# One PSUM copy per group product, joined by a DMA and GpSimd, in a float32 attention and MLP kernel

## The reference, cut to what matters

```
# q, k, v: (2, 8, 768, 64)   proj: (64, 6)
q_bits = (einsum('bhsd,dk->bhsk', q, proj) > 0)          # k_bits likewise
q_bucket = sum(q_bits * 2 ** arange(6), axis=-1)
mask = q_bucket[..., :, None] == k_bucket[..., None, :]
scores = where(mask, q @ k.T / 8, -1e9)
attn = exp(scores - max(scores)); attn = attn / (sum(attn) + 1e-9)
x = (attn @ v) transposed to (1536 tokens, 512)
h = x @ w_in1;  x = (P(h) / (Q(h) + 1e-6)) @ w_out1      # d_ff 2048, P cubic, Q quadratic
h = x @ w_in2;  out = (h - tanh(h)) @ w_out2
```

## Time and profile before

| | |
|---|---|
| time, median of 3 runs | 791.07 us (790.76 to 792.19) |
| the profiled execution's own time | 794.7 us |
| its span, first to last instruction | 792.9 us |
| TensorE busy | 771.3 us, 97% |
| VectorE busy | 554.0 us, 70% |
| ScalarE busy | 476.0 us, 60% |
| GpSimd busy | 127.3 us, 16% |
| mean granted TensorE clock | 0.993 of full speed |

### The profile page before, as it was taken

How to read it: one execution, slowest core, us unless ns; L and a number is a source line. 1 busy time by engine, 2 the same in 40 slices (tenths; PEclk the granted TensorE clock), 3 DMA queues, 4 the chain that set the end, 5 groups by cost and what they waited for, 6 DMA issues and landing times.

```text
span 792.9 us, 11860 instructions
## 1 busy us (share of the span) xinstructions
PE 771.3 (97%) x3840; PEld 645.7 (81%) x3840; DVE 554.0 (70%) x894; ACT 476.0 (60%) x922; POOL 127.3 (16%) x112
## 2 busy tenths in 40 slices
PE   5979999999999999999999999999999999999998
PEld 3879899989998777877888888888888888888886
DVE  4859999999997999999888988965432322223222
ACT  5859889888887778887666767654432222222221
POOL 5334533543548200000000000000000000000000
PEclk9989999999999999999999999999999999999999
DMA  5766768768563520000000032330000100001001
GB/s 116 157 167 154 163 163 175 172 152 175 120 171 114 159 94 0 1 2 1 0 1 15 26 107 83 103 92 3 0 1 1 53 1 1 0 1 54 0 1 54
DMA packets 64603, 56.54 MB, mean 71 GB/s; under 512 B 31664, under 2 KB 50352, under 8 KB 64560
## 3 DMA queue, kind: packets, MB, share of 16 engines
q1 hardware_dynamic: 62848, 55.52, 28.4%
q10 hardware_dynamic: 1712, 0.46, 0.3%
HBM read 29.57 MB, written 3.19 MB: 41 GB/s over the span
## 4 chain that ended last, share of the span: by engine, by line
PE 75%; DVE 16%; issue 3%; DMA 2%; POOL 2%; SPq 1%; ACT 1%; DVEq 0%; POOLq 0%; ACTq 0%
PE acc L722 28%; PE h_ps L693 27%; PE slot L232 5%; PE turn_ps L354 5%; PE pv_ps L314 4%; PE pv_ps L316 3%; DVE sqr L828 2%; DVE row_min L505 2%; DVE pol L849 2%; DVE pol L841 1%; DVE pt_lo L552 1%; DVE pol L860 1%; DVE pol L835 1%; DVE wout_lo L889 1%; DVE g_lo L873 1%
## 5 line engine op out<-in xcount | busy, mean ns | idle before, releaser
L693 PE MATMUL h_ps<-x_hi,win_lo 128*128 128x512 f32 x384 | 151.6, 395 | 0.0
L693 PE MATMUL h_ps<-x_lo,win_hi 128*128 128x512 f32 x384 | 151.4, 394 | 0.0
L693 PE MATMUL h_ps<-x_hi,win_hi 128*128 128x512 f32 x384 | 151.2, 394 | 0.0
L743 ACT ACTIVATE g_hi<-pol 128x512 fp32r<-128x512 f32 x96 | 60.8, 634 | 129.5 <-PE acc L722 105.2
L873 DVE TENSOR_TENSOR g_lo<-pol,g_hi 128x512 fp32r<-128x512 f32 x96 | 65.9, 687 | 101.2 <-ACT g_hi L743 101.0
L552 DVE TENSOR_TENSOR pt_lo<-turn_ps,pt_hi 128x384 fp32r<-128x384 f32 x192 | 98.0, 551 | 11.2 <-ACT pt_hi L457 9.6
L457 ACT ACTIVATE pt_hi<-turn_ps 128x384 fp32r<-128x384 f32 x192 | 84.0, 490 | 23.7 <-PE turn_ps L354 22.7
L505 DVE TENSOR_REDUCE row_min<-slot 128x1 f32<-128x768 f32 x96 | 90.7, 944 | 7.1 <-PE slot L232 7.1
L433 ACT ACTIVATE E<-slot,row_min 128x768 f32<-128x768 f32 x96 | 87.3, 909 | 2.8 <-DVE row_min L505 2.8
L693 PEld LDWEIGHTS h_ps<-x_lo,win_hi 128*128 128x128 f32 x384 | 72.2, 188 | 17.0
L693 PEld LDWEIGHTS h_ps<-x_hi,win_hi 128*128 128x128 f32 x384 | 72.2, 188 | 16.7
(11 more groups left out here) (105 smaller groups left out, 1364.9 us busy)
## 6 DMA issues: line engine op xcount, KB each, us to landing
win_raw<-in_moe_w_in SPq DMA_DIRECT2D x32, 256.0 KB, 3.1
wout_raw<-in_moe_w_out SPq DMA_DIRECT2D x32, 256.0 KB, 2.8
q_nat<-in_q SPq DMA_DIRECT2D x16, 192.0 KB, 3.5
v_nat<-in_v SPq DMA_DIRECT2D x8, 384.0 KB, 5.4
scale<-softmax_scale SPq DMA_DIRECT2D x16, 192.0 KB, 3.3
qA<-q_hi SPq DMA_DIRECT2D x15, 192.0 KB, 2.5
qB<-q_hi SPq DMA_DIRECT2D x15, 192.0 KB, 2.9
qB<-q_lo SPq DMA_DIRECT2D x15, 192.0 KB, 3.2
```

The lines of the kernel that those rows point to most:

```text
L693: mm = eng.matmul(h_ps[t % 4][:, :], w[:, ws], columns(x, kt, c), start=kt + n == 0, stop=kt == KT - 1 and n == 2)
L743: eng.activation(g_hi[:, t % TEMPS, :], pol[:, t % TEMPS, :], ACT.Copy).then_inc(mlp_sems["g_hi"], 1)
```

## The change

- v's parts are placed so that head e's result always has its hi product on the partitions where head e's x belongs: hi in columns 64e to 64e+63, lo in the other half.
- One copy takes all 128 partitions of `pv_ps` to a new tile `x_raw[e]`: ScalarE for groups 0, 2 and 3, VectorE for group 1. The next group's product waits for that copy only.
- A new DMA per head, `shift`, moves the 64 rows of `x_raw[e]` that lie on the wrong partitions into `x_pair` (64 rows of 768 float32, 192 KB). A new GpSimd add, `pool_add`, adds the other 64 rows. A copy out waits until the same half of `x_raw` was added in the pair before.
- SyncE: shift(p-1, 1) stands between copy_split(p+1, 0) and scale_out(p, 0). scale_in(p, 0) moves behind copy_hot(p+1, 1), and shift(p, 0) follows it.
- GpSimd: pool_add(p, 0) stands in step 11, behind the split of q and ahead of that of k; pool_add(p-1, 1) stands in front of the multiply of `pool_x`. Of the weight tiles, two are split ahead of the last pair's steps and the others behind them, in the order in3, in4 after in2 with the `out` tiles between.
- The one-hot products alternate: q half 0, k half 0, q half 1, k half 1. `dve_scale` of head 0 moves from step 4 to step 5.

```diff
-        POOL_TILES = ([("in", j) for j in range(EARLY_IN)] + [("out", j) for j in range(EARLY_OUT)]
-                      + LATE[:3])
+        POOL_TILES = [("in", 0), ("in", 1), ("in", 2), ("in", 3), ("out", 0), ("in", 4), ("out", 1),
+                      ("out", 2), ("in", 5)]
+        POOL_FIRST = 2
-        HOT_STEPS = {1: (0, 0), 2: (0, 1), 3: (1, 0), 4: (1, 1)}
+        HOT_STEPS = {1: (0, 0), 2: (1, 0), 3: (0, 1), 4: (1, 1)}
+        DVE_GROUP = 1
...
@@ def pe_pv
-                eng.wait_ge(sems["x_sum"], BIAS + GROUPS * p + c)
+                done, count = group_out(p, c - 1) if c else group_out(p - 1, GROUPS - 1)
+                eng.wait_ge(done, count)
...
-        def act_pv_low(eng, p, c):
+        def group_free(eng, p, c):
             eng.wait_ge(sems["pv"], BIAS + GROUPS * p + c + 1)
-            eng.wait_ge(sems["x_sum"], BIAS + GROUPS * p + c)
-            eng.activation(pv_low[:, :], pv_ps[D:2 * D, 0:HALF], ACT.Copy
-                           ).then_inc(sems["pv_low"], 1)
+            eng.wait_ge(sems["x_add"], BIAS + 2 * p - 1 + c // 2)
+
+        def act_out(eng, p, c):
+            if c != DVE_GROUP:
+                group_free(eng, p, c)
+                eng.activation(group_at(c), pv_ps[:, 0:HALF], ACT.Copy).then_inc(sems["out_act"], 1)
...
-        def dve_x_sum(eng, p, c):
-            e, hf = divmod(c, 2)
-            eng.wait_ge(sems["pv_low"], BIAS + GROUPS * p + c + 1)
-            if c == 0:
-                eng.wait_ge(sems["xn"], BIAS + p)
-            eng.tensor_tensor(x_pair[e * D:(e + 1) * D, hf * HALF:(hf + 1) * HALF],
-                              pv_ps[0:D, 0:HALF], pv_low[:, :], ALU.add
-                              ).then_inc(sems["x_sum"], 1)
+        def dve_out(eng, p, c):
+            if c == DVE_GROUP:
+                group_free(eng, p, c)
+                eng.tensor_copy(group_at(c), pv_ps[:, 0:HALF]).then_inc(sems["out_dve"], 1)
...
+        def pool_add(eng, p, e):
+            mine = slice(e * D, (e + 1) * D)
+            for c in (2 * e, 2 * e + 1):
+                done, count = group_out(p, c)
+                eng.wait_ge(done, count)
+            eng.wait_ge(loads[f"shift{e}"], 16 * (p + 1))
+            eng.sem_inc(loads["pool_here"], 1)
+            eng.tensor_tensor(x_pair[mine, :], x_pair[mine, :], x_raw[e][mine, :], ALU.add
+                              ).then_inc(sems["x_add"], 1)
...
@@ def pool_att
+            if last:
+                pool_split_tiles(eng, range(POOL_FIRST))
...
                 if n == 10 and turn:
                     pool_split_qk(eng, p + 2, 0)
+                if n == 11 and not last:
+                    pool_add(eng, p, 0)
             if last:
+                pool_split_tiles(eng, range(POOL_FIRST, len(POOL_TILES)))
+                pool_add(eng, p, 0)
+                pool_x(eng, p, sems["x_add"], BIAS + 2 * p + 1)
...
@@ SyncE
+                def shift(p, e):
+                    for c in (2 * e, 2 * e + 1):
+                        done, count = group_out(p, c)
+                        eng.wait_ge(done, count)
+                        here()
+                    eng.wait_ge(sems["xn"], BIAS + p)
+                    here()
+                    eng.dma_start(x_pair[e * D:(e + 1) * D, :], x_raw[e][D - e * D:2 * D - e * D, :]
+                                  ).then_inc(loads[f"shift{e}"], 16)
...
                     copy_split(p + 1, 0)
+                    if not is_zero(p):
+                        shift(p - 1, 1)
                     scale_out(p, 0)
                     load_v(p + 1)
                     copy_hot(p + 1, 0)
-                    scale_in(p, 0)
                     copy_split(p + 1, 1)
                     copy_hot(p + 1, 1)
+                    scale_in(p, 0)
+                    shift(p, 0)
                     scale_out(p, 1)
                     scale_in(p, 1)
...
@@ the last pair: weights, then
+                shift(PAIRS - 1, 0)
                 scale_out(PAIRS - 1, 1)
                 scale_in(PAIRS - 1, 1)
+                shift(PAIRS - 1, 1)
```

More of the change, by code:

```diff
@@ L67, in build @@
         "pe": ["pt", "pv", "scores0", "scores1", "aux"],
-        "act": ["pt_hi", "exp0", "exp1", "aux_act", "pv_low"],
-        "dve": ["rowmin", "sum", "recip", "aux_dve", "pt_lo", "x_sum"],
-        "pool": ["hi", "lo", "vhi0", "vhi1", "vlo0", "vlo1", "xn", "xhi", "xlo"],
+        "act": ["pt_hi", "exp0", "exp1", "aux_act", "out_act"],
+        "dve": ["rowmin", "sum", "recip", "aux_dve", "pt_lo", "out_dve"],
+        "pool": ["hi", "lo", "vhi0", "vhi1", "vlo0", "vlo1", "x_add", "xn", "xhi", "xlo"],
     }
@@ L143, in build @@
         row_inv = sb(att, "row_inv", [P, 2, T], F32)
-        pv_low = sb(att, "pv_low", [D, HALF], F32)
+        x_raw = [sb(att, f"x_raw{e}", [P, S], F32) for e in range(2)]
         x_pair = sb(att, "x_pair", [P, S], F32)
@@ L213, in exp_done, with group_out @@
             return sems[f"exp{m % 2}"], BIAS + p * T + m // 2 + 1
+        DVE_GROUP = 1
+        def group_out(p, c):
+            if c == DVE_GROUP:
+                return sems["out_dve"], BIAS + p + 1
+            return sems["out_act"], BIAS + (GROUPS - 1) * p + (c if c < DVE_GROUP else c - 1) + 1
         def is_zero(p):
@@ L260, in pe_hot @@
                 eng.wait_ge(sems["aux_dve"], dve_dot(b))
[L261 to L264, removed]
+            elif x == 1:
+                eng.wait_ge(sems["aux_dve"], dve_hot(b, h))
             else:
@@ L555, in dve_att @@
                                       ).then_inc(sems["pt_lo"], 1)
-                if n in (4, 9 if last else 10):
+                if n in (5, 9 if last else 10):
                     dve_scale(eng, p, n // T)
@@ L559, in dve_att @@
                     dve_step(eng, 0)
-                if last and n == TILES - 2:
-                    dve_x_sum(eng, p, GROUPS - 2)
                 if first and n == 2:
@@ L610, in x_slice, with pool_x @@
             return flat[:, bass.ds((p % PB) * TOK + (p // PB) * S, S)]
-        def pool_x(eng, p):
+        def pool_add(eng, p, e):
[7 more added lines that the diff above has]
+                              ).then_inc(sems["x_add"], 1)
+        def pool_x(eng, p, done, count):
+            eng.wait_ge(done, count)
+            pool_add(eng, p, 1)
             by_tile = lambda t: t.rearrange("m (t r) -> m t r", t=T)
-            eng.wait_ge(sems["x_sum"], BIAS + GROUPS * (p + 1))
+            eng.wait_ge(sems["x_add"], BIAS + 2 * (p + 1))
             for e in range(2):
@@ L665, in pool_split_weights, with pool_split_tiles @@
                               ).then_inc(mlp_sems["early_lo"], 1)
+        def pool_split_tiles(eng, numbers):
+            for i in numbers:
+                kind, j = POOL_TILES[i]
+                if kind == "in":
+                    pool_split_weights(eng, loads[f"w_in{j}"], w_in_slot[j], i)
+                else:
+                    pool_split_weights(eng, loads[f"w_out{j}"], w_out_slot[j], i)
         def split_in_count(layer, j):
@@ L1075, in _ @@
                     load_weight(0, "out", j)
+                shift(PAIRS - 2, 1)
                 scale_out(PAIRS - 1, 0)
```

37 lines of the change are left out of this document (18 added, 19 removed).

## The result

The changed kernel takes 795.44 us (median of 8 runs, 793.49 to 798.62) against 792.32 us for the kernel before on the same chip: a ratio of 1.0045, 95% interval 1.0024 to 1.0067. It is slower, by about what was forecast (793.1 against 791.07, a ratio of 1.0026). Behind the sum stand two terms that were both off.

A forecast was written before the change was run, and what follows sets the result against it. TensorE, busy 97% of the span, bounds the kernel, so only its waits could be won. Attention -0.2 us and handover +2.2 made +2.0: median 791.07 to 793.1 us, forecast band 791.9 to 795.5, full range 787.0 to 797.5.

The forecast's parts named there:

- Part 1: Attention, taking the products out: full copies replace half copies and sums; gain 0.4 us a pair, between 0 and 1.09.
- the one-hot order costs nothing: Order of the one-hot products in the attention steps: alternating them was said to cost nothing by itself.
- Part 2: GpSimd between the splits of q and k: `pool_add` delays head 0's operand copies in full, 1.9 us.
- Part 3: SyncE's burst of operand copies: the shift adds 0.94 us; with the add, operands 2.8 us later, stall 0.55 us in balance.
- so the engines, not SyncE, set the length: Burst of DMA copies: pair 0's 13.4 us against pair 3's 12.75 taken as showing this; crowding may add 0.65.
- dve_scale one step later: Softmax reciprocal of head 0: costs nothing by itself, as it comes near the time SyncE reaches `scale_out`.
- Part 4: From the last attention product to x_lo: two GpSimd adds delay the multiply and block VectorE; loss 2.2 us, bounds 0 and 5.5.
- The first two weight tiles are split in time that GpSimd has free: GpSimd before step 3 of pair 7: free time covers these splits; otherwise they would hold v's split, needed in step 9.
- The bound of 0: Handover, lowest loss: 0 us if GpSimd, not VectorE, is the one to wait each time.
- The fall of the granted clock: After a stall, a sign of being wrong: it would make the time worse than any bound given; no size.
- the transfers stay hidden: Rival for attention: operands only 1.7 us late, attention wins 4 to 7 us, handover takes 1 to 2; 787 us, chance 0.27.

The follow-up runs named there:

- a_add_late: Changed kernel with head 0's `pool_add` moved from step 11 to behind the split of k in the next pair's step 0; 796.10 us, ratio 1.0051.
- a_scale4: Changed kernel with `dve_scale` of half 0 (the reciprocal) back at step 4 instead of step 5; 795.38 us, ratio 1.0042.
- a_old_tail: Changed kernel with pair 6's groups 2 and 3 and pair 7 by half copy and sum, no early weight tiles, reciprocal at step 4; 791.87 us, ratio 0.9996.
- a_best_hot: Changed kernel with old end of attention, no early weight tiles, reciprocal at step 4, head 0's `pool_add` behind k's split, old one-hot order; 789.67 us, ratio 0.9968.
- a_shift_behind: Changed kernel with the previous pair's half 1 shift issued behind the first two one-hot copies instead of ahead of `scale_out`; 805.40 us, ratio 1.0169.
- b_two_adds: Kernel before with two extra 64x768 GpSimd adds ahead of the last pair's multiply; 793.60 us, ratio 1.0024.
- b_memsets: Kernel before with four GpSimd memsets of the 128x768 `x_norm` tile ahead of the last pair's multiply; 795.58 us, ratio 1.0045.

## Why the prediction was right, and where it was wrong

**Part 1, the copies.** Right in kind, low in size. The waits of the earlier trace rows are gone, ScalarE's copy took 0.496 us for a forecast 0.500. Forecast 0.4 us a pair, "nearer to the end where the old pace of VectorE remains"; pairs without a stall are 0.6 shorter (27.97, 27.99), and 0.8 with the old one-hot order and the reciprocal at its old step (27.79). That the one-hot order costs nothing was wrong for the kernel before, 0.55 us a pair; once the sum is gone 0.06 is left of it (27.85 against 27.79).

**Part 2, GpSimd's add.** Right: 1.84 us against 1.9, and the operands' copies start 1.94 later in pair 3 and 1.5 to 1.9 in pairs 4 to 6. In pair 2, behind the stall of pair 1, they start only 0.15 later: a stall gives time back to the next pair, as the forecast had it.

**Part 3, the shift.** Wrong: the forecast charged 0.94 us. The burst got no longer (12.6 against 12.75), so the delay at landing was 1.8 in pair 3, not 2.8. "so the engines, not SyncE, set the length" is the step that failed; the pause before `scale_out` could take the shift. What the shift's bytes cost in a burst without a pause, no run here shows. A TensorE that is faster by 0.6 needs the operands earlier, so a stall was left: 0, 0.36, 0 and 0.14 us in pairs 2 to 5 (0, 0.46, 0 and 0.8 in the second profile) against a forecast 0.55, and about 1 in pair 6 (periods 26.81 and 27.03, against 25.76 in a_add_late without a stall).

**dve_scale one step later.** Wrong: "the reciprocal then comes near the time at which SyncE, now later, reaches scale_out" holds from pair 3 on. In pair 1 the copies start before GpSimd's add can delay them, SyncE is at `scale_out` early, and stands there:

```profile
63.13 0.46 SPq L1063 DMA_DIRECT2D x_pair<-x_raw  x1
66.32 0.33 SPq L1044 DMA_DIRECT2D softmax_scale<-row_inv  x1
```

`k_hot` follows at 68.36 and lands 7.2 us later, in pair 2, after the same pause, 4.7. The stall of 2.3 us is this landing (7.2, 7.3 and 7.2 us in three executions). It goes when the reciprocal comes a step earlier (a_scale4), but also with the reciprocal and the pause as they are (a_add_late, landing after 3.4 us), so the step is not shown to be its cause, only one thing that can remove it; why the landing is slow stays open. I had put 0.2 us of gain on this pair, and it lost 1.6. The step also costs plain pairs 0.13 us, where I had nothing.

**Part 4, the handover.** Right in kind (the multiply starts 5.56 us later, and six VectorE instructions take 1.6 to 2.3 us in place of 0.7), too small in size: 2.2 forecast, 4.2 to 4.6 measured, within the bounds of 0 and 5.5. The mis-sized term is the start of the multiply. I had `pool_add(7, 0)` at 258 as the times ran before the change, 4.8 us after the last tile; it came at 8.5. "The first two weight tiles are split in time that GpSimd has free" failed: the split of in0 waited 2.58 us for its load, and v's split with all behind it came 5 us later after the pair's start (11.9 against 6.8). That used up the idle 5.14 us which should have covered the adds. a_old_tail, which takes out adds and early tiles, gives the 4 us back; the early tiles were never taken out alone, so how the 4 us divide between them and the adds is not shown (taking out the second add alone gave 1.4). That "GpSimd held something that they share" was my reading of two rows. What the runs show is the length of instructions beside each other: VectorE's `sqr` took 1.47 us beside an add and 0.75 beside a memset. The bound of 0 had GpSimd as the one to wait each time, and there both came out longer: GpSimd's adds took 2.29 and 2.02 us at the handover, against 1.84 at 235.55. The fall of the granted clock, named as what would make it worse, did come (0.52 from 274 to 276); what it cost, no run here shows. On balance -0.2 and +2.2 became -1.5 and 0.0 in two executions for attention from pair 1 on, and +4.6 and +4.2 for the rest; pair 0, which the forecast left out, moves by up to 3.8 us from one execution of the kernel before to the next, and the times of that kernel spread from 790 to 794.5. The total fits better than its parts, which is partly luck: part 3's charge was too high, part 4's too low, and pair 1 and pair 0 were not foreseen.

**The rivals.** For attention the truth lay between the forecast and "the transfers stay hidden"; a kernel with the new copies, the old end, the old one-hot order, the old step of the reciprocal and a later `pool_add` (a_best_hot) is the only one that is faster, by 0.3%, where that rival had 0.5.

## What to carry to other kernels

When work moves to an idle engine, cost its place in that engine's list and not its duration: 1.8 us of GpSimd add between two splits, or a wait for a DMA ahead of them, reached TensorE by way of SyncE's list, the DMA queue and VectorE (in pair 3 of the changed kernel the copies began 1.94 us later, the last landed 1.8 us later, and TensorE waited 0.33 us; a_shift_behind, with its wait of 12.15 us, took 10 us more). Before two tiles are split "for free", look when their load lands. And try each part of a bundled change alone: here one part (the copies) was worth having, one (the one-hots in turns) was a loss by itself, and small delays that the forecast had each put at nothing (the reciprocal's step, the two early tiles) show in the rows with 0.13 us a pair and a wait of 2.58 us.

## What the runs showed of the hardware

- In the changed kernel TensorE's granted clock fell to 0.52 to 0.63 after an idle time of 3.45 us at the handover, and 266 to 300 had a mean of 0.95; with b_two_adds (3.47 us idle) it was 0.95 too. In b_memsets, after 3.31 us idle, the same window kept 1.00. The length of one idle stretch does not tell it: a little earlier the changed kernel idled 2.44 us (until 263.01) and kept 1.00 from 264 to 268, and its second execution idled 2.14 us (until 264.22) and had 0.50 from 266 to 268.
- GpSimd's casts came out longer as well: in the changed kernel a 128x512 weight cast took 1.08 us at 252.71 and 255.10, beside VectorE instructions with two SBUF inputs, and 0.61 at 250.78, beside `pt_lo`, which has one input in PSUM.
- One transfer of 192 KB (`kA<-k_hot`), by the same queue, landed 4.0 to 7.2 us after its issue within one execution of the changed kernel; in pair 1 it took 7.2, 7.3 and 7.2 us in three executions with the same code up to there, and 3.4 in a_add_late.
